# The gate of a fused retention and feed-forward kernel: Silu on ScalarE becomes Sigmoid on ScalarE and a multiply on VectorE

## The reference

```
state = gamma * state + k^T v ; y = scale * q state        (8 heads of 64, retention)

rms = sqrt(mean(x * x) + 1e-6) ; xn = x / rms * rms_g      (gated layer, d_ff = 1536)
g = xn @ w_gate ; silu = g * (1 / (1 + exp(-g)))
x = (silu * (xn @ w_val)) @ w_out

p = domain_probs / (sum + 1e-9)                            (four experts, 1024 wide each)
out = sum over e of p[:, e] * (max(x @ w1[e], 0) @ w2[e])
```

## Time and profile before

| | |
|---|---|
| median of three runs | 861.85 us (860.26 to 863.49) |
| the profiled execution | 863.49 us |
| its span, first to last instruction | 861.7 us |
| PE busy | 838.0 us, 97% |
| PE weight loads busy | 774.7 us, 90% |
| DVE busy | 502.1 us, 58%, 787 instructions |
| ACT busy | 238.9 us, 28%, 482 instructions |
| POOL busy | 419.1 us, 49% |
| granted TensorE clock, mean | 0.992 |

### The profile page before, as it was taken

How to read it: one execution, slowest core, us unless ns; L and a number is a source line. 1 busy time by engine, 2 the same in 40 slices (tenths; PEclk the granted TensorE clock), 3 DMA queues, 4 the chain that set the end, 5 groups by cost and what they waited for, 6 DMA issues and landing times.

```text
span 861.7 us, 12795 instructions
## 1 busy us (share of the span) xinstructions
PE 838.0 (97%) x4836; PEld 774.7 (90%) x4836; DVE 502.1 (58%) x787; ACT 238.9 (28%) x482; POOL 419.1 (49%) x444
## 2 busy tenths in 40 slices
PE   8978999999999999899999999999999999999998
PEld 7757999999999999889898989998989899989897
DVE  3797755656565656795545455454554554545545
ACT  2546322233222323342222122222222222222221
POOL 3996683818182746773663254245336236336100
PEclk9998999999999999899999999999999999999999
DMA  9901000101011010100201101101101101110003
GB/s 338 338 24 49 24 26 24 50 25 50 25 33 42 25 49 25 50 0 2 74 25 50 49 1 50 49 1 49 49 0 49 49 5 47 49 37 14 26 6 141
DMA packets 12876, 43.58 MB, mean 51 GB/s; under 512 B 1553, under 2 KB 1553, under 8 KB 12817
## 3 DMA queue, kind: packets, MB, share of 16 engines
q1 hardware_dynamic: 12816, 42.77, 13.9%
HBM read 39.62 MB, written 3.15 MB: 50 GB/s over the span
## 4 chain that ended last, share of the span: by engine, by line
PE 87%; POOL 4%; DVE 4%; DMA 1%; issue 1%; ACT 1%; SPq 1%; DVEq 0%; POOLq 0%
PE bank L495 28%; PE bank L494 28%; PE bank L493 28%; DMA w_raw<-wu 1%; POOL w_raw L314 1%; POOL w_lo L337 1%; DVE x_sum L233 1%; POOL x_lo L237 1%; PE bank L472 1%; POOL squares L311 1%; DVE x_all L856 1%; PE bank L430 1%; DVE h_lo L914 1%; POOL w_hi L330 0%; DVE h_lo L920 0%
## 5 line engine op out<-in xcount | busy, mean ns | idle before, releaser
L493 PE MATMUL bank<-x_hi,w_hi 128*128 128x384 f32 x784 | 265.7, 339 | 6.1 <-ACT m L684 3.2
L494 PE MATMUL bank<-x_hi,w_lo 128*128 128x384 f32 x784 | 264.5, 337 | 0.0
L495 PE MATMUL bank<-x_lo,w_hi 128*128 128x384 f32 x784 | 264.5, 337 | 0.0
L961 DVE SCALAR_TENSOR_TENSOR out_acc<-bank,p_norm,out_acc 128x512 f32<-128x512 f32 x180 | 134.9, 750 | 127.6 <-PE bank L495 127.2
L493 PEld LDWEIGHTS bank<-x_hi,w_hi 128*128 128x128 f32 x784 | 148.6, 190 | 13.8 <-issue 7.8
L494 PEld LDWEIGHTS bank<-x_hi,w_lo 128*128 128x128 f32 x784 | 148.6, 190 | 5.6 <-issue 0.3
L495 PE MATMUL bank<-wd_lo,h_hi 128*128 128x512 f32 x384 | 151.7, 395 | 0.0
L494 PE MATMUL bank<-wd_hi,h_lo 128*128 128x512 f32 x384 | 151.2, 394 | 0.0
L493 PE MATMUL bank<-wd_hi,h_hi 128*128 128x512 f32 x384 | 149.3, 389 | 0.3 <-DVE out_acc L957 0.3
L495 PEld LDWEIGHTS bank<-x_lo,w_hi 128*128 128x128 f32 x784 | 148.4, 189 | 0.0
L337 POOL TENSOR_TENSOR w_lo<-w_raw,w_hi 128x256 fp32r<-128x256 f32 x196 | 145.1, 776 | 2.3
(11 more groups left out here) (69 smaller groups left out, 901.0 us busy)
## 6 DMA issues: line engine op xcount, KB each, us to landing
w_raw<-wu SPq DMA_DIRECT2D x28, 512.0 KB, 4.3
ring<-qkv SPq DMA_DIRECT2D x24, 512.0 KB, 8.7
wd_raw<-wd SPq DMA_DIRECT2D x22, 512.0 KB, 3.5
out<-out_acc SPq DMA_DIRECT2D x12, 256.0 KB, 2.0
decay_mask<-t_decay_mask SPq DMA_DIRECT2D x1, 512.0 KB, 6.0
y_decay<-t_y_decay SPq DMA_DIRECT2D x1, 256.0 KB, 7.7
small_sb<-small SPq DMA_DIRECT2D x1, 32.0 KB, 4.3
```

What stands on the lines that cost most here:

```text
L493: pe.matmul(dst, s_hi, m_hi, start=first, stop=False, skip_group_check=True)
L494: pe.matmul(dst, s_lo, m_hi, start=False, stop=False, skip_group_check=True)
L495: return pe.matmul(dst, s_hi, m_lo, start=False, stop=last, skip_group_check=True)
L961: nc.vector.scalar_tensor_tensor(out=to, in0=new, scalar=p, in1=to, op0=ALU.mult, op1=ALU.add).then_inc(posted, 1)
```

## The change

ScalarE computes Sigmoid instead of Silu, from the same banks into the same tile `gate`, and the table set loaded ahead is that of Sigmoid. A new VectorE operation `gated(q, a)` multiplies the gate columns, still in PSUM, by `gate`, in place. What waited for `silu_ready` (the hidden products, and TensorE's reuse of banks) now waits for `gated_ready`, which VectorE raises; `sig_ready` goes from ScalarE to VectorE. There are 24 units with two multiplies each, 48 in all.

```diff
             def sigmoid(q, a):
                 s = q % 2
                 if a == 0:
                     act.wait_ge(c11_ready, q + 1)
-                    nc.scalar.activation(gate[:, s, 0, :], bank[3 * s + 2][:, 0:TB], ACT.Silu).then_inc(silu_ready, 1)
+                    nc.scalar.activation(gate[:, s, 0, :], bank[3 * s + 2][:, 0:TB], ACT.Sigmoid).then_inc(sig_ready, 1)
...
-            nc.scalar.preload_act_table_set("silu_and_others")
+            nc.scalar.preload_act_table_set("sigmoid_and_others")
...
+            def gated(q, a):
+
+                s = q % 2
+                dve.wait_ge(sig_ready, 2 * q + a + 1)
+                nc.vector.tensor_tensor(gate[:, s, a, :], bank[3 * s + (0 if a else 2)][:, 0:TB], gate[:, s, a, :],
+                                        ALU.mult).then_inc(gated_ready, 1)
+
             def hidden(q, a):
                 s, slot = q % 2, q % SLOTS1
-                dve.wait_ge(silu_ready, 2 * q + a + 1)
+                dve.wait_ge(gated_ready, 2 * q + a + 1)
...
                 c11(q)
                 some(1)
+                gated(q, 0)
                 c22_sum(q)
                 some(2)
+                gated(q, 1)
                 hidden_all(q)
...
             part_lo(1, "S1")
+            gated(0, 0)
+            gated(0, 1)
             hidden(0, 1)
             c12(0)
             hidden(0, 0)
             c11(1)
             c22_sum(1)
             part_lo(1, "S2")
+            gated(1, 0)
+            gated(1, 1)
             hidden(1, 1)
...
             c11(q)
+            gated(q, 0)
             c22_sum(q)
             post1(end, 0, 3)
+            gated(q, 1)
             hidden(q, 1)
```

More of the change, by code:

```diff
@@ L199, in build @@
         c12_ready = sem("c12_ready")
-        silu_ready = sem("silu_ready")
+        gated_ready = sem("gated_ready")
+        sig_ready = sem("sig_ready")
         hid_ready = sem("hid_ready")
@@ L507, in product @@
                 if name == "M1" and 2 <= q < Q1 + 2:
-                    pe.wait_ge(silu_ready, 2 * (q - 2) + 2)
+                    pe.wait_ge(gated_ready, 2 * (q - 2) + 2)
                 elif name == "M1" and q >= Q1 + 2:
@@ L515, in product @@
                 elif name == "M2" and 2 <= q < Q1 + 2:
-                    pe.wait_ge(silu_ready, 2 * (q - 2) + 1)
+                    pe.wait_ge(gated_ready, 2 * (q - 2) + 1)
                 elif name == "M2" and q >= Q1 + 2:
@@ L545, in tile1 @@
                 elif i in (2, 4):
-                    pe.wait_ge(silu_ready, 2 * Q1 if i == 2 else 2 * Q1 - 1)
+                    pe.wait_ge(gated_ready, 2 * Q1 if i == 2 else 2 * Q1 - 1)
                 elif i == 3:
@@ L684, in copy_up, with sigmoid @@
                 nc.scalar.activation(tile[:, s, :], bank[3 * s][:, 0:TB], ACT.Copy).then_inc(u_copied, 1)
-            def silu(q, a):
+            def sigmoid(q, a):
                 s = q % 2
@@ L689, in silu @@
                     act.wait_ge(c11_ready, q + 1)
-                    nc.scalar.activation(gate[:, s, 0, :], bank[3 * s + 2][:, 0:TB], ACT.Silu).then_inc(silu_ready, 1)
+                    nc.scalar.activation(gate[:, s, 0, :], bank[3 * s + 2][:, 0:TB], ACT.Sigmoid).then_inc(sig_ready, 1)
                 else:
                     act.wait_ge(up_done, up_count(q, "M4"))
-                    nc.scalar.activation(gate[:, s, 1, :], bank[3 * s][:, 0:TB], ACT.Silu).then_inc(silu_ready, 1)
+                    nc.scalar.activation(gate[:, s, 1, :], bank[3 * s][:, 0:TB], ACT.Sigmoid).then_inc(sig_ready, 1)
             def hidden_hi(q, a):
@@ L704, in unit1 @@
                 copy_up(q, "M6", u2)
-                silu(q, 0)
+                sigmoid(q, 0)
                 copy_up(q, "M7", u3)
-                silu(q, 1)
+                sigmoid(q, 1)
                 hidden_hi(q, 1)
@@ L757, in _ @@
             copy_up(0, "M6", u2)
-            nc.scalar.preload_act_table_set("silu_and_others")
+            nc.scalar.preload_act_table_set("sigmoid_and_others")
             copy_up(0, "M7", u3)
-            silu(0, 0)
-            silu(0, 1)
+            sigmoid(0, 0)
+            sigmoid(0, 1)
             copy_up(1, "M1", m1)
@@ L770, in _ @@
             hidden_hi(0, 0)
-            silu(1, 0)
-            silu(1, 1)
+            sigmoid(1, 0)
+            sigmoid(1, 1)
             hidden_hi(1, 1)
```

## The result

| | before | changed |
|---|---|---|
| median of seven runs | 862.39 us (860.26 to 865.09) | 867.40 us (865.47 to 868.95) |
| profiled execution | 863.49 us | 866.84 us |
| its span | 861.7 us | 864.7 us |

The ratio is 1.0057, 95% interval 1.0042 to 1.0072: the changed kernel is slower by about 5.0 us. The forecast was 866.4 us, slower by 0.53% of the median then shown; the range 862.5 to 870.0 holds the result.

What follows compares the result with a forecast made beforehand. TensorE was taken to set the time, so VectorE work costs only where TensorE waits. 3.2 us in the layer plus 1.3 in the opening made 4.5 over the median 861.85: 866.4 us, range 862.5 to 870.0.

Steps and rivals of the forecast that it cites:

- Costs nothing: Gated layer: Sigmoid at 492 ns, table load at 1.28 us, and 24 first multiplies fitting VectorE's 1.08 us idle add nothing.
- Quiet units: Units 5, 9, 13, 17, 21: 1.4 us of slack before the tile covers the added 0.6 us; even units also free.
- Units 7, 11, 15, 19: GpSimd holds VectorE's product and low parts, making the next output tile 0.8 us late, four times: 3.2 us (2.7 to 3.2).
- the walk: Unit 7 step by step: the last low part ends near 161.05 instead of 160.26, 0.8 us late.
- the four waits that were to be seen: Sign: TensorE waits of about 1 us for low parts before the tiles after units 7, 11, 15, 19.
- second walk: Unit 7 with GpSimd starting 0.4 us later, held up by unit 6: last low part ends at 160.93, costing 0.67.
- Unit 3: Its low parts end 0.3 us early and its product already waits for GpSimd as long as the multiply lasts: nothing.
- The opening: Units 0 to 2: four multiplies in VectorE's packed stretch delay the first output tile by 1.05 or 1.7, taken as 1.3 us.
- Rival 1: Opening: TensorE's clock falls to half level after its wait, adding 2.7 us, 869.1 us; chance 15%.
- Rival 2: Even units: the product loses the port to w_hi and waits 1.7 us longer, unit 22's M1 copy 1.3 late: 867.7 us; 15%.
- Rival 3: End of the gated layer: VectorE's last low part gets the port before GpSimd, returning 1.5 us: 864.9 us; chance 15%.

Runs made afterwards that it cites:

- small GpSimd: GpSimd's sums and splits of up weights in blocks 4 to 11 cut to one column: 861.69 us under the kernel before, 864.76 us under the changed one.
- the four: Changed kernel keeping only the second multiplies of units 7, 11, 15 and 19, Sigmoid alone elsewhere: 865.43 us, 1.0035 to the kernel before.
- units 0 and 1: Changed kernel with multiplies only in its first two units, Sigmoid alone elsewhere: 864.82 us, 1.0037 to the kernel before.
- units 2 to 23: Changed kernel with multiplies left out in its first two units, Sigmoid alone there: 865.92 us, 1.0051 to the kernel before.
- the rest: Changed kernel with 44 multiplies, the second ones of units 7, 11, 15 and 19 left out: 865.26 us, 1.0036 to the kernel before.

## Why the prediction held, point by point

- **Costs nothing: Sigmoid, its table, the first multiply.** Shown by the run without multiplies (1.0000) and, for the first multiply in its own unit, by the stretch with the small GpSimd (1212 of 1213). With GpSimd at its full work the multiplies other than the four did cost the layer 1.1 us.
- **Quiet units free.** Shown for their own tiles: no wait in units 6, 10, 14, 18, 22.
- **Units 7, 11, 15, 19, 3.2 us.** The mechanism was right, and the walk's size too when the four multiplies are alone (3.1 to 3.2 us; the last low part ends at 161.05, as walked). In the changed kernel it is 2.6 us: the term was too large by 0.6. The step that fails is "four times". The four places now wait 0.18, 0.57, 1.06 and 1.08 us, so one of the four waits that were to be seen, that after unit 7, is not there: GpSimd came later than walked, and the low parts fell between its sums. In unit 15 GpSimd is 0.35 us late, close to the second walk, but the place costs 1.0 us and not 0.67. The prediction named the M1 copy behind the first product but gave it no price; it is 0.4 us of the waits in units 16 and 20. The waits also differ between executions of the same order (2.4 to 3.0 us), so the 2.6 is one draw.
- **Unit 3 free.** Nearly: 0.12 us in unit 4.
- **The opening, 1.3 us.** In the chain 1.1 us, at the lower of the two ends that were given: the last low part did get in ahead of GpSimd. The M6 of unit 2 was put 2.2 us later (90.45 less 88.24), and is 2.6 less the 0.46 of the later start, 2.2.
- **Rival 1, the clock.** It was given 15% as a case of its own, at 2.7 us. Four of six profiles with this wait show it, at 1.5 us: ten matmuls at 0.32 us, where the rows that gave the price had nineteen. By the mean clock it is worth 0.8 us over the executions of this kernel. This is a mis-sized chance, and a large part of what the forecast lacked.
- **Outside the span, 0.35 us.** No term of the prediction. All kernels with the whole set of 48 multiplies show it and the others, with up to 44, do not; what it is stays open.
- **Rival 2, even units.** The race was as close as worked out (0.05 us) and was won in all six units. It was not a matter of chance: product and w_hi keep the same 0.05 us from unit 6 on in every profile with these multiplies.
- **Rival 3, the end of the layer.** The order stayed: 1.8 us of wait, as before. That the order is worth about 1.4 us is shown by the run that turns it round.
- **The sum.** 1.1 for the chain of the opening, 1.9 to 2.6 for the layer, 0.35 outside the span and 0.8 to 1.0 for the clock make about 4.2 to 5.1; measured 5.0. The forecast of 4.5 had 0.2 and 0.6 too much in its two terms and lacked the other two, 1.2 to 1.4, so its closeness is partly luck.
- **Why the halves do not add up.** The medians of units 0 and 1 and of units 2 to 23 (+2.5 and +3.6 us) make 6.1, those of the four and the rest (+3.3 and +3.2) 6.5, while the whole costs 5.0. The traces show where most of it is: the layer is longer by 3.5 us with units 2 to 23 alone, by 3.2 with the four and 1.1 with the rest, but by 2.6 with all. Each is one profile, and a median has an interval of about 1.3 us either way, so the last few tenths stay open.

## What to carry to other kernels

Work on an engine with 40% idle time is not free and not priced by its length: look where its results are due, and price it there. Look also at what it does to the other engines' start times: here a multiply in a unit with slack made GpSimd late, and that cost something a unit later. Where two engines share a way into SBUF, ask at each due place which instruction of the other engine will be under way when the moved one comes; a whole instruction of 1.7 us can be waited out, however small the shift was. And count what stands behind in the queue: in three of the moves here the wait went to the next instruction of the same queue.

## What the runs showed of the hardware

- A multiply with one PSUM and one SBUF operand is not held by GpSimd: all 48 took 540 to 558 ns, and 17 of them ran wholly while GpSimd was at work, while the product with two SBUF operands has a mean of 802 ns and up to 1.44 us. The Trainium skill, "SBUF — State Buffer", section "Who interferes with whom", says so, and the trace agrees.
- The order at the port is settled by 0.05 us: the product at 237.93 against w_hi at 237.98 was not held (0.56 us), and w_hi took 2.07 us instead of 1.70.
- After a wait of TensorE of 2.2 us the clock fell to its half level in four of six executions, which cost 1.5 us; after 3.0 us, before M6 of unit 24, in twelve of fourteen. After waits of 1.8 us before the tile at the end of the layer, and of up to 1.1 us in the layer, it stayed at 1.00 in all of them; so it did after the three of 2.0 to 2.45 us at other matmuls of the opening.
